# Attention's weight work, head casts and tail copies moved by a step, its last steps reordered, and some zero matmuls on 64 rows

## What is computed

```python
rel = pos[:, None] - pos[None, :]
scores = scale * (q @ k.T)
scores = where((rel >= 0) & (rel < 128), scores - slopes * abs(rel), -1e9)
attn = exp(scores - max(scores)); attn = attn / (sum(attn) + 1e-9)
x = (attn @ v), heads side by side        # 2304 x 512, float32
h = x @ w_in                               # 512 x 2048
x = (h * sigmoid(1.702 * h)) @ w_out       # 2048 x 512
h = x @ w_in2
g = where(h >= 1, h, where(h <= -1, 0, (h + 1) ** 2 / 4))
out = g @ w_out2
```

## Time and profile before

| | |
|---|---|
| median of three runs | 871.19 us (870.68 to 871.20) |
| the profiled execution, its own time | 870.5 us |
| its span, first to last instruction | 868.7 us |
| PE busy | 851.5 us, 98% of the span |
| DVE, ACT, POOL busy | 713.5, 537.4, 115.2 us |
| mean granted clock of PE | 0.998 of full |

### The profile page before, as it was taken

One profiled execution on the slowest core, in us unless ns is written; L12 is line 12 of the kernel. 1 busy time (PEld: TensorE's weight loads), 2 busy tenths in 40 slices (PEclk: granted clock), 3 DMA queues, 4 the chain that ended last, 5 costly groups with the idle time before them and its releaser, 6 DMA issues.

```text
span 868.7 us, 15510 instructions
## 1 busy us (share of the span) xinstructions
PE 851.5 (98%) x5746; PEld 845.4 (97%) x5746; DVE 713.5 (82%) x984; ACT 537.4 (62%) x788; POOL 115.2 (13%) x81
## 2 busy tenths in 40 slices
PE   7999999999999999999999999999999999999998
PEld 7999889999999999999999999999999999999998
DVE  7889897577798868677997988898989779889784
ACT  5887778576774545676744555767556467765441
POOL 4787788000000000000000000000000000000000
PEclk9999999999999999999999999999999999999999
DMA  8876951568667265587775664488556643888822
GB/s 191 214 206 186 241 151 67 189 233 307 219 206 278 97 255 192 210 316 252 266 242 219 243 231 161 135 307 295 195 194 220 229 156 146 290 287 303 307 75 73
DMA packets 63241, 186.45 MB, mean 215 GB/s; under 512 B 7488, under 2 KB 14336, under 8 KB 59328
## 3 DMA queue, kind: packets, MB, share of 16 engines
q1 hardware_dynamic: 63168, 185.46, 63.0%
HBM read 113.09 MB, written 72.35 MB: 213 GB/s over the span
## 4 chain that ended last, share of the span: by engine, by line
PE 87%; DVE 6%; POOL 3%; issue 3%; ACT 1%; DVEq 0%; POOLq 0%; ACTq 0%
PE ps L1053 80%; PE ps L1021 3%; PE ps L987 2%; DVE qk_hi L1533 2%; PE ps L1000 1%; DVE probs L1557 1%; POOL qk_hi L893 1%; POOL k_lo L889 1%; DVE wst L1590 1%; PE ps L1030 0%; PE ps L1015 0%; DVE heads_out L1570 0%; DVE w_first L1603 0%; POOL qk_raw L933 0%; POOL wst L903 0%
## 5 line engine op out<-in xcount | busy, mean ns | idle before, releaser
L1053 PE MATMUL ps<-arena,w_first 128*128 128x384 f32 x1764 | 331.5, 336 | 0.9 <-ACT ps L1305 0.8
L1053 PEld LDWEIGHTS ps<-arena,w_first 128*128 128x128 f32 x1764 | 310.7, 188 | 2.4 <-issue 1.7
L1053 PE MATMUL ps<-arena,w_rest 128*128 128x384 f32 x1260 | 240.8, 337 | 0.9 <-ACT ps L1305 0.8
L1053 PEld LDWEIGHTS ps<-arena,w_rest 128*128 128x128 f32 x1260 | 220.1, 188 | 2.0 <-issue 1.7
L1661 DVE TENSOR_TENSOR arena<-raw_first,arena 128x768 fp32r<-128x768 f32 (+1 forms) x114 | 148.8, 1318 | 78.0 <-ACT arena L1272 78.0
L1272 ACT ACTIVATE arena<-raw_first 128x768 fp32r<-128x768 f32 (+1 forms) x120 | 132.0, 1117 | 45.6 <-DVE raw_first L1619 39.1
L1053 PE MATMUL ps<-w_rest,arena 128*128 128x256 f32 x945 | 132.4, 281 | 0.0
L1053 PEld LDWEIGHTS ps<-w_rest,arena 128*128 128x128 f32 x945 | 121.1, 189 | 0.1
L1053 PE MATMUL ps<-w_first,arena 128*128 128x256 f32 x567 | 88.0, 282 | 0.0
L1661 DVE TENSOR_TENSOR arena<-raw_rest,arena 128x1536 fp32r<-128x1536 f32 (+1 forms) x48 | 71.3, 1486 | 11.6 <-ACT arena L1272 11.5
L1053 PEld LDWEIGHTS ps<-w_first,arena 128*128 128x128 f32 x567 | 76.0, 189 | 0.0
(11 more groups left out here) (116 smaller groups left out, 971.8 us busy)
## 6 DMA issues: line engine op xcount, KB each, us to landing
gd<-g SPq DMA_DIRECT2D x24, 1536.0 KB, 6.1
raw_rest<-gd SPq DMA_DIRECT2D x32, 768.0 KB, 5.1
wst<-w_pairs SPq DMA_DIRECT2D x32, 512.0 KB, 6.1
raw_first<-gd SPq DMA_DIRECT2D x16, 768.0 KB, 6.2
yd<-ust SPq DMA_DIRECT2D x6, 1536.0 KB, 6.3
qk_raw<-qkT SPq DMA_DIRECT2D x30, 288.0 KB, 4.4
wd<-ust SPq DMA_DIRECT2D x4, 1536.0 KB, 9.4
raw_first<-yd SPq DMA_DIRECT2D x4, 1536.0 KB, 7.8
```

The costliest lines, as they stand in the source:

```text
L1053: last = nc.tensor.matmul(to, stationary, moving, start=start and n == 0, stop=n == len(steps) - 1, skip_group_check=True)
```

## The change

It has five parts.

1. The tail of a pair is transposed (PE) one step sooner, in step 2 behind the transposition of probabilities, and not in step 3. It is copied by ACT in step 3 and not by DVE in step 4. Only the last pair's tail copy stays with DVE.
2. DVE casts the odd head in step 1 and not in step 2, and does its weight work in step 2, behind the tails' bias, and not in step 1. Some of ACT's roundings move by one or two steps with it.
3. At the end of attention, the mark of bank 3 moves from `duo` into step 82 and signals with bank 4's mark a new semaphore that ACT's `seed_b` waits for. In the first `duo`, the first product_6 stands ahead of the last pair's transposition and not behind it.
4. ACT copies the last pair behind `copy_d`, not before it.
5. Three quarters of the zeros' matmuls of `warm_up` take 64 rows and not 128, the last half of them alternating between the upper and the lower rows, and into another bank.

```diff
-PAIR_TAIL_LAG = 9
-COPY_TAIL_LAG = 10
+PAIR_TAIL_LAG = 8
+COPY_TAIL_LAG = 9
-CAST_LAG = (2, 3)
+CAST_LAG = (2, 2)
...
-            for _ in range(count):
-                nc.tensor.matmul(ps[:, 5, 0:BAND], arena[:, 0:P], arena[:, P:P + BAND], start=True, stop=True)
+            for n in range(count):
+                rows = (slice(0, P), slice(0, DIM), slice(0, P), slice(DIM, P))[n % 4 if n < count // 2 else 1 + 2 * (n % 2)]
+                nc.tensor.matmul(ps[:, 6 if rows.start else 5, 0:BAND], arena[rows, 0:P], arena[rows, P:P + BAND], start=True, stop=True)
...
+        def mark_first_b():
+            pe.wait_ge(pt_copied[0], 2 * PAIR_COUNT)
+            mark_written(3).then_inc(banks_marked, 1)
...
             else:
-                for bank in range(2):
-                    pe.wait_ge(pt_copied[bank], 2 * PAIR_COUNT)
-                mark_written(3)
+                pe.wait_ge(pt_copied[1], 2 * PAIR_COUNT)
                 product_5(u, up, c, k, D, 0)
+                product_6(u, up, c, k, D, 0)
                 transpose_pair(PAIR_COUNT - 1)
                 mark_written(5)
                 mark_written(6)
-                product_6(u, up, c, k, D, 0)
                 product_5(u, up, c, k, D, 1)
...
+        def copy_pair_tail(q):
+            pair = q % BATCH_PAIRS
+            act.wait_ge(pair_tail_transposed, q + 1)
+            for half in range(2):
+                rows = slice(half * TAIL, (half + 1) * TAIL)
+                last = nc.scalar.activation(x_pairs[rows, pair, 4 * P:SEQ], xt_bank[rows, rows], ACT.Copy)
+            last.then_inc(pair_tail_copied, 1)
...
+            if (q := pair_at(m, COPY_TAIL_LAG)) is not None:
+                copy_pair_tail(q)
-            if m in (32, 53):
-                round_weights((32, 53).index(m), 1)
-            if m in (44, 62, 67, 69, 77, 79):
-                round_operand(0, (44, 62, 67, 69, 77, 79).index(m))
+            if m in (32, 54):
+                round_weights((32, 54).index(m), 1)
+            if m in (44, 64, 69, 70, 77, 79):
+                round_operand(0, (44, 64, 69, 70, 77, 79).index(m))
...
-            if m in (41, 71):
-                split_last_weights(0 if m == 41 else 1)
-            if m in (46, 51):
-                add_weights(1, (0,) if m == 46 else (1, 2))
-            if m in (61, 66):
-                sum_operand(0, S1 if m == 61 else S2)
-            if m in (76, ALL_STEPS):
-                add_weights(2, (0,) if m == 76 else (1, 2))
+            if m in (42, 72):
+                split_last_weights(0 if m == 42 else 1)
+            if m in (47, 52):
+                add_weights(1, (0,) if m == 47 else (1, 2))
+            if m in (62, 67):
+                sum_operand(0, S1 if m == 62 else S2)
+            if m in (77, ALL_STEPS):
+                add_weights(2, (0,) if m == 77 else (1, 2))
```

More of the change, by code:

```diff
@@ L218, in build @@
     lo_made = sem("lo_made")
+    banks_marked = sem("banks_marked")
     p1_done = sem("p1_done")
@@ L1057, in mark_written @@
         def mark_written(bank):
-            nc.tensor.matmul(ps[:, bank], operand(0, A11)[:, 0, 0, 0:P],
-                             w_place(0)[:, 0].rearrange("p h n -> p (h n)"), start=True, stop=True)
+            return nc.tensor.matmul(ps[:, bank], operand(0, A11)[:, 0, 0, 0:P],
+                                    w_place(0)[:, 0].rearrange("p h n -> p (h n)"), start=True, stop=True)
         def weights_ready(w):
@@ L1129, in first_product_1 @@
                 pe.wait_ge(scores_biased, ALL_STEPS)
-                mark_written(4)
+                mark_written(4).then_inc(banks_marked, 1)
             product_1(0, True, 0, 0, 0, n)
+        def mark_first_b():
+            pe.wait_ge(pt_copied[0], 2 * PAIR_COUNT)
+            mark_written(3).then_inc(banks_marked, 1)
         def duo(u, up, c, k, D):
@@ L1180, in _ @@
                 first_product_1(m - ALL_STEPS)
+            if m == ALL_STEPS + 2:
+                mark_first_b()
         for u in range(PHASES):
@@ L1277, in _ @@
         make_bias(0)
-        for m in range(ALL_STEPS + TRANSPOSE_LAG):
+        for m in range(ALL_STEPS + DRAIN):
             for gi, (_, last_step) in enumerate(GROUPS):
@@ L1301, in seed_b @@
             if D == 0:
-                act.wait_ge(p5_done, 1)
+                act.wait_ge(banks_marked, 2)
             wait_past(act, c11_out, D)
@@ L1392, in up @@
             seed_b(D, 1)
-            if D == 0:
-                copy_pair(PAIR_COUNT - 1)
             if c == 0 and u:
@@ L1397, in up @@
             copy_d(D, 0)
+            if D == 0:
+                copy_pair(PAIR_COUNT - 1)
             if k:
@@ L1571, in write_pair, with copy_last_tail @@
                                     at.unsqueeze(3).to_broadcast([P, 2, SLOTS // 2, DIM]), ALU.mult).then_inc(pair_written, 1)
-        def copy_pair_tail(q):
-            pair = q % BATCH_PAIRS
-            dve.wait_ge(pair_tail_transposed, q + 1)
+        def copy_last_tail():
+            dve.wait_ge(pair_tail_transposed, PAIR_COUNT)
             for half in range(2):
                 rows = slice(half * TAIL, (half + 1) * TAIL)
-                last = nc.vector.tensor_copy(x_pairs[rows, pair, 4 * P:SEQ], xt_bank[rows, rows])
+                last = nc.vector.tensor_copy(x_pairs[rows, BATCH_PAIRS - 1, 4 * P:SEQ], xt_bank[rows, rows])
             last.then_inc(pair_tail_copied, 1)
@@ L1633, in _ @@
         round_first(0)
-        for m in range(ALL_STEPS + COPY_TAIL_LAG - 1):
+        for m in range(ALL_STEPS + WRITE_LAG):
             if (q := pair_at(m, WRITE_LAG)) is not None:
@@ L1654, in _ @@
                     round_head(head)
-            if (q := pair_at(m, COPY_TAIL_LAG)) is not None:
-                copy_pair_tail(q)
         def split_operand(k, i):
@@ L1779, in up @@
                 if k == 0:
-                    copy_pair_tail(PAIR_COUNT - 1)
+                    copy_last_tail()
                 add_weights(w + (3 if u < 2 else 4))
```

## The result

| | before | after |
|---|---|---|
| median | 871.20 us (870.68 to 871.52, four runs) | 878.97 us (878.67 to 879.78, four runs) |
| span of the profiled execution, its own time | 868.7, 870.5 us | 876.9, 878.67 us |

A forecast was written before the change was run, and what follows sets the result against it. It took rounds 2 to 7 as bound by PE, 8 to 14 mostly by DVE. Terms 3.5 - 0.3 + 1.7 + 0.9 - 0.5 + 0.3 = +5.6 us gave a forecast median of 876.8 us, range 870.0 to 880.5.

The forecast's parts named there:

- The tail's transposition a step sooner: Rounds 2 to 7, 11 and 15: PE's tail transposition waits for ACT's copy_pair, +3.5 us, bounds 1.5 and 5.
- DVE's relief: Tail copies leave DVE's queue, but the time is mostly lost waiting for POOL: -0.3 us, bounds 0 and -3.3.
- Head 20 late: Around round 8's weight work: SP's weight load issues 1.8 us later, DVE waits some 2.7 for head 20; +1.7 us.
- rival E: Longer waits in rounds 9 and 10 bring a second or longer fall of the granted clock: 878.5 to 881, chance 0.08.
- Round 10: Three of DVE's instructions meet POOL there, not two: one more wait, +0.9 us, bounds 0 and 1.4.
- The same sum after; nothing is gained: Rounds with one piece of weight work: swapped cast and weight work still meet POOL, 1.76 + 1.69 before and after.
- The end: End of attention: product_6 ahead of the last pair's transposition covers PE's wait of 0.42 us; -0.5, bounds -0.6 and 0.
- The zeros: Warm-up matmuls on 64 rows ahead of the scores: only a later clock rise could cost; +0.3 us, bounds -0.2 and 1.3.
- as long: Warm-up zeros: if 64-row matmuls take the same time as 128-row ones, nothing changes.
- two at once: Warm-up zeros: if two run together, PE idles before the scores; a later clock rise would add about 1 us.

The follow-up runs named there:

- tails_only: The kernel before with only the tails' part: tail transposed in step 2, copied by ACT in step 3; 871.75 us, ratio 1.0012.
- tails_copy_first: The kernel of tails_only with ACT's copy_pair ahead of the exponentials of its step, not behind them; 868.99 us, ratio 0.9971.
- act_copy_only: The kernel before with the tail still transposed in step 3, only its copy moved from DVE to the head of ACT's step 4; 868.20 us, ratio 0.9964.
- zeros_only: The kernel before with only the new zeros' matmuls of the change; 875.20 us, ratio 1.0051.
- weights_only: The kernel before with only the casts and the weight work in each other's place, with ACT's roundings; 873.41 us, ratio 1.0029.
- after_old_zeros: The changed kernel with the zeros' matmuls as before; 874.15 us, ratio 1.0036.
- mended: The kernel of copy_end_load with, besides, casts and weight work where the change puts them; 867.65 us, ratio 0.9958.
- copy_end_load: The kernel before with tail copy on ACT in step 4, reordered end of attention, and weight 2's load behind heads 20 and 21; 867.39 us, ratio 0.9961.
- weights_load_later: The kernel of weights_only with SP's load of weight 2 behind the loads of heads 20 and 21, not ahead; 869.20 us, ratio 0.9981.
- zeros_one_half: The kernel before with all 38 zeros' matmuls on 64 rows, all on the upper half of the array; 872.60 us, ratio 1.0015.
- zeros_two_halves: The kernel before with all 38 zeros' matmuls on 64 rows, halves in turn, each half into its own bank; 871.59 us, ratio 1.0001.

## Why the forecast was right in sign, and where its sum was off

The forecast of 876.8 lay 2.2 below the time, inside its range. Two terms were wrong in opposite directions, by +3.8 and -2.5, and the total hides it: that it came so near is luck.

1. **The tail's transposition a step sooner, +3.5: right.** Rounds 2 to 7 measured +3.5 in the changed kernel and in tails_only, for my 2.95 (1.25 and 1.39 in round 2, 0.4 and 0.5 in rounds 3 to 6). The 0.1 a round that I missed is the transposition's own start-up behind a wait: its row lasts 0.33, not 0.27 as in the earlier trace rows; that reading is argued, not tested. The other 0.6 of my term, for rounds 11 and 15, can't be seen apart there. tails_copy_first shows that in rounds 2 to 7 the wait was the whole cost; in time the two kernels lie 2.7 apart, since the rounds from 8 on give part of it back.
2. **DVE's relief, -0.3 of 0 to -3.3: mis-sized, it measured -2.8** (act_copy_only). I took the end of the bounds at which POOL swallows all of it. That happens in round 8. But the meeting of two engines is not only a price that DVE can't escape: started earlier, it can miss the meeting. The Trainium skill's exclusive lock (SBUF — State Buffer, "SBUF: two separate sides": of two instructions the one that starts first has the shared ports to its end) fits both orders in round 13, 2.19 for the cast that comes second and 0.76 for the one that comes first; I had read it for one sign of an effect that has two. The 2.8 is not a clock fall less, though act_copy_only's trace has none: on the same chip five runs of the kernel before with a granted clock of 1.000 have a median of 871.03, and the four such runs of act_copy_only lie between 867.79 and 868.40. In zeros_only, which has no fall either, rounds 11 and 12 together are only 0.34 shorter, so a fall in round 11 is mostly paid back.
3. **Head 20 late, +1.7: right in mechanism, too small in size.** SP's issue came 0.03 behind the weight work and DVE waited 3.22 and 3.03 (2.7 expected). The price was higher: round 9 was 3.35 longer, with PE's wait and the clock fall behind it, and putting the load in time took 4.2 off weights_only, where my upper bound was 2.2. The clock fall is rival E's mechanism, but it replaced the one of round 11, instead of coming on top, so the changed kernel has one fall as before. That the fall costs the whole kernel anything isn't shown: after_old_zeros takes as long in its two runs without one.
4. **Round 10, +0.9: right, measured 0.5 to 0.7** (mended against copy_end_load; weights_load_later). In the changed kernel the odd head's cast takes 1.52 and the two pieces of weight work 2.90, for 0.75 and 2.78 before: 0.9 more of DVE's time, as expected.
5. "The same sum after; nothing is gained": **wrong**, rounds 13 and 14 are 1.65 shorter in weights_only. That the whole part measured 2.4, near the 1.7 + 0.9 of terms 3 and 4, is luck: this gain stands against a load that cost more. Round 15 gives 1.0 of that back, as it does in every kernel that gained there: PE then waits for POOL's subtraction of the last heads, in act_copy_only so:

```profile
138.55 0.38 PE L987 MATMUL ps<-qk_hi 128*128 128x256 f32 x1 [0.73 <-POOL qk_hi L893]
```

6. **The end, -0.5**: measured -0.7, with an interval that reaches just over nothing.
7. **The zeros, +0.3 of -0.2 to 1.3: the step that failed; it measured +4.1.** I weighed only "as long" and "two at once". The third case, that a matmul of one shape behind one of another costs more than either, I didn't price, though the diff alternates shapes in 18 places. Of the 4.18, 1.06 is the clock's late rise (zeros_one_half, within my bound), and the other 3.1, the distance between that kernel and this one, the exchanges, less what running side by side gives back.

With the measured terms the sum would be 3.5 - 2.8 + 2.4 - 0.7 + 4.1 = 6.5, for 7.8 measured. Of the 1.3 between, 0.9 is there with the old zeros too; the table shows where it can come from. In rounds 13 and 14 the two parts miss their sum by 1.8, of which round 15 returns 0.9, since its wait for POOL is paid once and not twice; in rounds 11 and 12 they miss it by 1.0, of which 0.34 is the fall that neither has. The traces can't be brought closer to the medians, since that of weights_only is 1.67 under its own; the other 0.4 is within the medians' scatter.

## What to carry to other kernels

Where an edit changes the shape or the placement of work that looks free, such as warm-up matmuls, price the transition from one to the next, not only each instruction; the queue of weight loads shows what a pipelined PE row hides. Price a relief from both sides: two engines that meet can also miss each other, and of two edits that shorten the same rounds only one is paid. And before moving an instruction that gates a transfer, look at what is queued behind that transfer: here one call moved in SP's queue turned 2.4 us of loss into 1.7 us of gain. It was worth nothing clear with the old places and the copies on ACT (copy_end_load), although DVE waited 1.3 us for the load there without it.

## What the chip showed that I had not expected

- Going from a 128-row to a 64-row matmul or back costs PE's weight loads 0.22 us idle, 18 times 0.22 in the changed kernel, each load then 0.51 behind the last; zeros_one_half and zeros_two_halves, with no such change among their 22, have no such idle. zeros_one_half has it once more, where its 64-row zeros follow the 128-row scores at 7.50, and the kernel before has none there. The Trainium skill says that changing the tiling mode drains TensorE (TensorEngine Tiling (Array Packing), "Key Properties"); the trace agrees, and gives the price.
- 64-row matmuls on alternating halves take 0.12 us each with 256 columns at the lower clock, half of the 0.23 of those on one half.
- After 22 matmuls of 128 rows in 5.06 us the scores' rows show the higher level from the second on; after 22 of 64 rows in the same 5.06 us, only from 16.1 us. In all ten traces with the old zeros the shorter rows are there by 7.6 us, in the four with zeros on 64 rows not before 16 (19.1 in the changed kernel). What in the half rows makes the difference was not tested.
